# A fused attention and two-layer MLP kernel on one core: weight remainders in halves and at other places, and attention stages in another order

## The reference

```python
# q, k, v: (4 batches, 8 heads, 576, 64)
q_d, k_d, v_d = means over groups of 4 positions
out_up = repeat(softmax(q_d k_d^T / 8) v_d, 4)
out_local = softmax(where(|i - j| < 4, q k^T / 8, -1e9)) v
x = (out_up + out_local) as (2304 tokens, 512)
x = (silu(x w_gate) * (x w_val)) w_out        # d_ff 1536
y = (relu(x w_in) ** 2) w_out2                # d_ff 2048
```

## Time and profile before

| | |
|---|---|
| runs | 945.2, 943.93, 942.46 us; median 943.93 |
| profiled execution | 945.5 us, its span 943.7 us |
| busy: PE, DVE, ACT, POOL | 915.8, 649.4, 403.7, 225.8 us |
| mean granted TensorE clock | 0.982 |
| attention alone | until 53.4 us |
| slots 0 to 47 with pass 0 | 53.4 us to about 242 us |
| passes 1 to 5 begin at | about 282, 421, 562, 704, 846 us |

### The profile page before, as it was taken

The page is one execution under the profiler, slowest core; times in us unless marked ns, Lnnn a source line. Parts: engine busy times, 40 slices in busy tenths (PEclk is TensorE's granted clock), DMA queues, the critical chain, the costliest instruction groups (busy, mean ns, idle before and its releaser), DMA issues.

```text
span 943.7 us, 17134 instructions
## 1 busy us (share of the span) xinstructions
PE 915.8 (97%) x6704; PEld 881.8 (93%) x6704; DVE 649.4 (69%) x1110; ACT 403.7 (43%) x733; POOL 225.8 (24%) x279
## 2 busy tenths in 40 slices
PE   6889999999999999999999999999999999999998
PEld 4678998998999999989999989999999999999998
DVE  6557555655287847696747598666788666778775
ACT  2445454545246443536443535232435232435231
POOL 5575454544242100231100133000323000302000
PEclk8589999999999999999999999999999999999999
DMA  6553333322231111321031121000232010211422
GB/s 198 174 175 93 104 91 103 105 68 73 81 113 49 53 34 34 96 87 49 30 108 53 60 90 67 1 18 17 82 101 71 17 51 17 79 59 54 135 68 67
DMA packets 70880, 71.36 MB, mean 76 GB/s; under 512 B 27280, under 2 KB 58000, under 8 KB 70800
## 3 DMA queue, kind: packets, MB, share of 16 engines
q1 hardware_dynamic: 68496, 65.55, 22.8%
q10 hardware_dynamic: 2304, 4.72, 1.3%
HBM read 56.10 MB, written 14.16 MB: 74 GB/s over the span
## 4 chain that ended last, share of the span: by engine, by line
PE 80%; DVE 9%; ACT 5%; issue 2%; SPq 1%; POOL 1%; DMA 0%; ACTq 0%; DVEq 0%
PE mlp_ps L929 11%; PE mlp_ps L930 10%; PE mlp_ps L931 10%; PE sc L929 5%; PE sc L930 5%; PE sc L931 5%; PE xp L930 4%; PE xp L929 4%; PE xp L931 4%; PE tr L788 3%; PE sd L929 2%; PE sd L931 2%; PE sd L930 2%; PE sc L769 2%; PE tr L929 2%
## 5 line engine op out<-in xcount | busy, mean ns | idle before, releaser
L1309 ACT ACTIVATE wh_hi<-hbuf 128x384 fp32r<-128x384 f32 x144 | 72.4, 524 | 85.4 <-DVE hbuf L1595 61.0
L689 POOL TENSOR_TENSOR w_raw<-w_raw 128x256 f32<-128x256 f32 x16 | 16.7, 1045 | 355.8 <-DMA w_raw<-w_in 355.8
L1603 DVE TENSOR_TENSOR wh_lo<-hbuf,wh_hi 128x384 fp32r<-128x384 f32 x144 | 76.0, 560 | 24.1 <-ACT wh_hi L1309 20.6
L1558 DVE TENSOR_TENSOR ring<-ring_raw,ring 128x768 fp32r<-128x768 f32 x96 | 90.3, 963 | 0.0
L1258 ACT ACTIVATE ring<-ring_raw 128x768 fp32r<-128x768 f32 x96 | 75.3, 836 | 28.9 <-DVE ring_raw L1552 28.6
L929 PE MATMUL mlp_ps<-ring,w_hi 128*128 128x384 f32 x240 | 80.6, 336 | 2.5 <-DVE vbuf L1571 1.9
L931 PE MATMUL mlp_ps<-ring,w_lo 128*128 128x384 f32 x240 | 80.2, 334 | 0.0
L930 PE MATMUL mlp_ps<-ring,w_hi 128*128 128x384 f32 x240 | 80.2, 334 | 0.0
L929 PE MATMUL mlp_ps<-wh_hi,w_hi 128*128 128x384 f32 x216 | 73.2, 339 | 2.6 <-DVE wh_lo L1603 1.5
L930 PE MATMUL mlp_ps<-wh_lo,w_hi 128*128 128x384 f32 x216 | 72.2, 334 | 0.0
L931 PE MATMUL sc<-wh_hi,w_lo 128*128 128x384 f32 x216 | 72.2, 334 | 0.0
(11 more groups left out here) (201 smaller groups left out, 2715.1 us busy)
## 6 DMA issues: line engine op xcount, KB each, us to landing
ring_raw<-x_whole SPq DMA_DIRECT2D x24, 384.0 KB, 3.6
ring_raw<-y_whole SPq DMA_DIRECT2D x24, 384.0 KB, 3.6
qk_sb<-qT SPq DMA_DIRECT2D x16, 288.0 KB, 2.9
qk_sb<-kT SPq DMA_DIRECT2D x16, 288.0 KB, 3.2
v_grp<-v SPq DMA_DIRECT2D x32, 144.0 KB
x_whole<-x_f ACTq DMA_DIRECT2D x16, 288.0 KB, 2.7
y_whole<-ypart SPq DMA_DIRECT2D x3, 1536.0 KB, 5.7
v_win<-v SPq DMA_DIRECT2D x64, 64.0 KB, 2.6
```

The costliest lines, as they stand in the source:

```text
L689: nc.gpsimd.tensor_tensor(block(5), block(7), block(4), ALU.add).then_inc(s_usum[i], 1)
L1309: nc.scalar.activation(hi[:, f, t, :], hbuf[:, e, :], ACT.Copy).then_inc(s_shhi, 1)
L1558: nc.vector.tensor_tensor(ring[:, SLOTS[g][p], 1, :, :], whole(g, p), ring[:, SLOTS[g][p], 0, :, :].bitcast(F32), ALU.subtract).then_inc(s ...
L1603: nc.vector.tensor_tensor(lo[:, f, t, :], hbuf[:, e, :], hi[:, f, t, :].bitcast(F32), ALU.subtract)\
```

## The change

- `SPLIT_IN`, `SPLIT_BEHIND` and `SPLIT_NEXT` become tables for ACT (`HI_...`) and for DVE (`LO_...`); DVE's name halves of a unit, and `LO_SUM` is a further place on DVE, between `dve_c11` and the hidden values of a group in the pass's first chunk.
- Product 2 of a new unit waits only for the first half of its remainder, product 5 for the second.
- Units 0 and 1 of the gated passes swap places in the weight buffer, and pass 0's first tile moves with them. Unit 0 of pass 3 then takes the place of unit 0 of pass 2, which is free earlier.
- Pass 0: DVE's stage 3 goes ahead of stage 7, save in the last slot of a batch. In a batch's first slot the last k step of both tiles comes behind the rest, and ACT's copy of the transposed local probabilities comes ahead of silu. The output tiles m = 0 and m = 1 are run in the order (0,0) (0,1) | (0,2) (1,0) | (1,1) (1,2) | (0,3) (1,3) over the four parts of two slots (tile, hidden tile), and DVE copies both out in the second slot.

```diff
-SPLIT_IN = {2: {2: [0], 3: [1]}, 3: {3: [0]}, 4: {2: [0]}, 5: {2: [0]}}
-SPLIT_BEHIND = {3: [1], 4: [1], 5: [1]}
-SPLIT_NEXT = {1: {0: [2], 1: [3]}, 2: {0: [2], 1: [3]}, 3: {0: [2]}, 4: {0: [2]}, 5: {}}
+HI_IN = {2: {2: [0]}, 3: {2: [0]}, 4: {2: [0]}, 5: {2: [0]}}
+HI_BEHIND = {2: [1, 2], 3: [1, 2], 4: [1, 2], 5: [1]}
+HI_NEXT = {1: {1: [3]}, 2: {0: [3]}}
+LO_IN = {2: {2: [(0, 0), (0, 1)]}, 3: {2: [(0, 0), (0, 1)]}}
+LO_BEHIND = {4: [(0, 0), (0, 1), (1, 0), (1, 1)], 5: [(0, 0), (0, 1), (1, 0), (1, 1)]}
+LO_SUM = {2: {0: [(1, 0), (1, 1)]}, 3: {0: [(1, 0), (1, 1)], 1: [(2, 1)]}, 4: {1: [(2, 1)]}}
+LO_NEXT = {1: {0: [(2, 0), (2, 1)], 1: [(3, 0), (3, 1)]}, 2: {0: [(2, 0), (2, 1)], 1: [(3, 0), (3, 1)]},
+           3: {0: [(2, 0)]}, 4: {0: [(2, 0)]}}
...
-UNITS = [[("in", f, [3072, 0, 1024, 2048][f], 2 * KT * P) for f in range(NF[0])]
+UNITS = [[("in", f, [5376, 0, 1024, 2048][f], 2 * KT * P) for f in range(NF[0])]
...
-    return ([5376, 3584, 0, 1792] if gated(ps) else [3584, 0, 1792])[i]
+    return ([3584, 5376, 0, 1792] if gated(ps) else [3584, 0, 1792])[i]
...
         def pe_mlp(pe, it, cp, j, part):
...
+            starts_batch = j == 0 and cp == 0 and it > 0
+            if j < NF[0] and not starts_batch:
+                pe_first_in(pe, it, cp, j, part, 0, KT)
+            elif j == 0:
+
+                pe_first_in(pe, it, cp, 0, part, 0, KT - 1)
+                if part:
+                    for tile in range(2):
+                        pe_first_in(pe, it, cp, 0, tile, KT - 1, KT)
+            elif it < BATCH - 1 and j < NF[0] + 2:
+
+                for m, f in (((0, 0), (0, 1)), ((0, 2), (1, 0)), ((1, 1), (1, 2)), ((0, 3), (1, 3)))\
+                        [2 * (j - NF[0]) + part]:
+                    pe_first_out(pe, it, cp, m, f, f + 1)
...
-            if c == 0 and p == 2:
-                pe.wait_ge(s_ulo[j], 2 * units_up_to(ps, j))
+            if c == 0 and p in (2, 5):
+
+                pe.wait_ge(s_ulo[j], 2 * units_up_to(ps, j) - (p == 2))
...
         def dve_slot(d, g):
+
+            ends_batch = g % BATCH_SLOTS == BATCH_SLOTS - 1
+            if not ends_batch:
+                for i in pairs_in(3, g):
+                    dve_normalise_loc(d, i)
             for i in pairs_in(7, g):
                 dve_sum_branches(d, i)
...
+            if c == 0:
+                for i, k in LO_SUM.get(ps, {}).get(j, []):
+                    dve_unit_lo(d, ps, i, k)
```

More of the change, by code:

```diff
@@ L933, in pe_mlp, with pe_first_in @@
         def pe_mlp(pe, it, cp, j, part):
-            order = bank_order(it)
+            starts_batch = j == 0 and cp == 0 and it > 0
[10 more added lines that the diff above has]
+                    pe_first_out(pe, it, cp, m, f, f + 1)
+            else:
+                pe_first_out(pe, it, cp, j - NF[0], part * NF[0] // 2, (part + 1) * NF[0] // 2)
+        def pe_first_in(pe, it, cp, j, part, k0, k1):
             c = 2 * it + cp
-            if j < NF[0]:
+            _, _, a, _ = UNITS[0][j]
+            pos = 2 * j + part
+            if k0 == 0:
                 if c == 0:
                     pe.wait_ge(s_firstlo[j], 1)
-                _, _, a, _ = UNITS[0][j]
-                pos = 2 * j + part
                 wait_bank(pe, it, cp, pos)
[L942 to L947, removed]
+            for k in range(k0, k1):
+                if j == 0 and part == 0:
+                    pe.wait_ge(s_xlo, 2 * (PAIRS * it + k) + cp + 1)
+                last = split_products(mlp_bank(it, pos), a + (k * 2 + part) * P,
+                                      (xin[:, x_slot(it, cp), 0, k, :], xin[:, x_slot(it, cp), 1, k, :]),
+                                      k == 0, k == KT - 1)
+            if k1 == KT:
                 last.then_inc(s_in if part else s_gate, 1)
-            else:
-                pe_first_out(pe, it, cp, j - NF[0], part * NF[0] // 2, (part + 1) * NF[0] // 2)
         def pe_first_out(pe, it, cp, m, f0, f1):
@@ L1176, in act_slot @@
                 act_move_ds(a, i, 1)
+            starts_batch = g > 0 and g % BATCH_SLOTS == 0
+            if starts_batch:
+                for i in pairs_in(4, g):
+                    act_move_loc1(a, i)
             act_mlp(a, *mlp, "gate")
@@ L1182, in act_slot @@
             for i in pairs_in(4, g):
-                act_move_loc1(a, i)
+                if not starts_batch:
+                    act_move_loc1(a, i)
                 act_move_loc2(a, i)
@@ L1366, in act_chunk @@
             if c == NC - 1 and ps + 1 < PASSES:
-                for i in SPLIT_BEHIND.get(ps + 1, []):
+                for i in HI_BEHIND.get(ps + 1, []):
                     act_unit_hi(a, ps + 1, i)
@@ L1495, in dve_slot @@
                 dve_maximum_ds(d, i)
-            for i in pairs_in(3, g):
-                dve_normalise_loc(d, i)
+            if ends_batch:
+                for i in pairs_in(3, g):
+                    dve_normalise_loc(d, i)
             for i in pairs_in(4, g):
@@ L1517, in dve_mlp @@
                 m = j - NF[0]
-                d.wait_ge(s_out, MT + out_tile(c, m) + 1)
-                nc.vector.tensor_copy(ypart_at(c, m), out_bank(it, m)).then_inc(s_y, 1)
+                for t in {0: [], 1: [0, 1]}.get(m, [m]) if it < BATCH - 1 else [m]:
+                    d.wait_ge(s_out, MT + out_tile(c, t) + 1)
+                    nc.vector.tensor_copy(ypart_at(c, t), out_bank(it, t)).then_inc(s_y, 1)
         def dve_hidden_lo(d, gi, lo, B, hi):
@@ L1638, in dve_group @@
             if c == NC - 1 and ps + 1 < PASSES:
-                for i in SPLIT_IN[ps + 1].get(j, []):
-                    dve_unit_lo(d, ps + 1, i)
+                for i, k in LO_IN.get(ps + 1, {}).get(j, []):
+                    dve_unit_lo(d, ps + 1, i, k)
             if c == 0:
-                for i in SPLIT_NEXT[ps].get(j, []):
-                    dve_unit_lo(d, ps, i)
+                for i, k in LO_NEXT.get(ps, {}).get(j, []):
+                    dve_unit_lo(d, ps, i, k)
         def dve_y(d, g, i):
@@ L1693, in dve_chunk @@
             if c == NC - 1 and ps + 1 < PASSES:
-                for i in SPLIT_BEHIND.get(ps + 1, []):
-                    dve_unit_lo(d, ps + 1, i)
+                for i, k in LO_BEHIND.get(ps + 1, []):
+                    dve_unit_lo(d, ps + 1, i, k)
             dve_y(d, g, 7)
@@ L1700, in dve_last_batch @@
             if cp == 0 and j == 4:
-                dve_unit_lo(d, 1, 0)
+                for k in range(2):
+                    dve_unit_lo(d, 1, 0, k)
             if cp == 0 and j == 5:
@@ L1720, in dve_last_batch @@
             if cp == 1 and j == 5:
-                dve_unit_lo(d, 1, 1)
+                for k in range(2):
+                    dve_unit_lo(d, 1, 1, k)
         def dve_mask(d):
```

18 lines of the change are left out of this document (8 added, 10 removed).

## The result

| | before | changed |
|---|---|---|
| runs beside each other, median | 943.74 us of 4 | 956.37 us of 4 (951.54 to 957.12) |
| ratio | | 1.0121, 95% interval 1.0093 to 1.0148 |
| profiled execution, its span | 945.5, 943.7 us | 957.12, 955.3 us |
| mean granted TensorE clock | 0.982 | 0.980 |

The changed kernel is slower, as forecast, but by 11.4 us by the ratio (by its interval 8.8 to 14.0; the two medians are 12.6 apart), where the sum said 6.2. It ends above the forecast's range, whose upper end was 954.5. A second session timed the same kernel at 954.05 against 944.54 of the kernel before (1.0101, 1.0085 to 1.0118), so 9 to 13 us are to be explained.

The account below looks back on a forecast made before the run. PE, busy 97% of the span, was taken as the bound. Parts 1 to 3 add 11.9 and part 4 takes off 5.75: +6.2 on 943.9 gives 950.1 us; the sum's ends are 945 and 953, the range 943.5 to 954.5.

Parts of the forecast that it names:

- Part 1: Pass 0, DVE normalises before summing: slots 11 to 35 lose 4 x 1.38, slots 7, 23, 39 lose 3 x 0.73.
- part 2: Batch starts, slots 16 and 32: transposition starts no earlier, three matmuls now behind it, 0.4 more each, 0.8.
- Rivals 1 and 2: Pass 0: ACT's chain stays hidden, 936.0, chance 0.08; or only branch-sum waits and batch starts cost, 939, chance 0.06.
- Slots 3 and 43: Pass 0, late coarse normalising: slot 3 loses 1.5 (1.3 to 1.8), slot 43, without slack, loses 1.9.
- Part 3: Pass 0, output tiles' new order: last hidden tile used some 2.5 us later, nothing further to count.
- Part 4: Pass changes, weight units' remainders moved: 5.75 us less in all, bounds 4 to 7.
- The same at the end of pass 2: Unit 0's remainder goes a group earlier there: gain 1.5, as at the end of pass 1.
- First groups of passes 3 and 4: PE's pauses there come from both halves of unit 2's remainder; moving one behind gains 0.7 each, 1.4.
- rival 3: As forecast, but moved remainders also late, at product 2 of passes 4 and 5 and first groups: +2.4, 952.5, chance 0.12.
- The first 60 us: Kernel start, where attention runs alone: only a place in memory changes, so no time gained or lost.

Follow-up runs that it names:

- gate_first: The changed kernel with ACT's gate silu ahead of the splits of x in slots 3, 11, 19, 27, 35 and 43: 941.21 us, ratio 0.9972.
- tiles_old: The changed kernel with output tiles 0 and 1 again in the old order, each copied out in its own slot: 954.31 us, ratio 1.0121.
- after_again: The changed kernel run once more with no edit: 954.05 us, ratio 1.0101 to the kernel before.
- lo21_back: Kernel before with only the new remainder tables and swapped places, unit 2's second half again in group 0 of passes 3 and 4: 938.39 us.
- pool_late: Kernel before with only the new remainder tables and swapped places, POOL's next-unit sums held back at the ends of passes 1 and 2: 942.22 us.
- gate_plain: lo21_back with ACT's gate silu first in slots 3, 11, 19, 27, 35 and 43: 937.83 us, ratio 0.9933.
- gate_tiles: gate_plain with the changed kernel's order of output tiles 0 and 1 besides: 939.99 us, ratio 0.9953.

## Why the prediction was wrong in its size

- **Part 1, slots 11 to 35 and 7, 23, 39; part 2: right.** 4 x 1.38 + 3 x 0.73 + 2 x 0.4 = 8.5 forecast, 4 x 1.28 + 2.4 + 0.8 = 8.3 measured, by the mechanism named. At the batch start the transposition starts no earlier and three matmuls stand behind it, as said. Rivals 1 and 2, in which this chain is hidden, have fallen with gate_first.
- **Slots 3 and 43, "I take 1.5" and 1.9: mis-sized, the largest error.** The chain alone costs 2.0 (tiles_old) and 1.8 (after_again). Behind pauses this long PE's clock fell to half, another 1.2 in slot 43; slot 3 shows 1.5 more, the fall and 0.3 or so of the tiles' order together. The sum had a pause's length and its refill and no price for the clock: 3.4 for the two slots against 6.5 in the profiled execution and 5.3 in the second.
- **Part 3, the output tiles, at nothing: right**, within 0.3 in slot 3 and nothing elsewhere. It names other waits (w_lo, buf_b, probsT_l), and the sum of the pauses stays.
- **Part 4, 5.75 less: too large, by 1.75.** "The same at the end of pass 2: 1.5" failed most: that end gave 0.4. The pause ahead of it went as forecast (1.2 with its refill), but the wait for wh_lo grew from 0.36 to 0.62, as POOL's sums stood beside both of DVE's products, and the wait for ypart behind it from 0.54 to 1.04, as POOL's sum there started ahead of DVE's copy. I had used the trace's 1.62 for two products beside POOL, and took pass 2's end to be like pass 1's. "First groups of passes 3 and 4, 0.7 each ... from both halves of unit 2's remainder, of which one is moved behind" failed in its cause and then in its size: by lo21_back the 0.4 that is gained comes from ACT's hi part being ready earlier, and moving the half gives 0.3 more and takes it back a group later. That is my rival 3 in kind (the moved remainders late), but not in place: at product 2 of passes 4 and 5, where I looked for it, nothing waits.
- **The first 60 us, at nothing.** The profiled execution of the changed kernel lost 0.9 there, its second gained 0.6: the execution's, not the change's.

Sum, of the profiled execution: 0.9 + (14.8 - 11.9) + (5.75 - 4.0) = 5.5, and its span is longer by 11.6, where the forecast had 6.2. In after_again it is -0.6 + 13.6 - 3.5 = 9.5, as its span is longer by 9.5. Both parts erred the same way, so no error hid another. (One slip besides: the chances of rivals 1 and 2 add up to 0.14, and "faster" was given 0.13.) By its sign and chain the forecast was right; its upper end of 953, in the sum, held no case in which a long pause costs more than itself.

## To carry to other kernels

Before an in-order engine's idle wait is filled with other work, list who waits for the work that used to fill it: here DVE's branch sums were ACT's ticket to the splits and the silu queued behind them, and putting silu first in that queue gave back 11 us by the steps of pass 0 (13 by the medians). In this kernel a pause of 2 to 3 us on a busy PE cost its length and, five times in eight, a stretch at half clock worth 1.2 to 1.4 us more; such a chance belongs in the sum. And an instruction moved out of a pause lands somewhere else; ask which engine works beside it there.

## What the hardware showed that I had not expected

- The half clock behind pauses of 2 to 3 us in all: in eight such places five had it and three did not, and slot 44 of the changed kernel had it in one execution of two. Each time it lasted 3.4 us, and cost 1.2 to 1.4 between like programs. Behind the single pauses of 1.9 us in pool_late (at 418.94 and 558.40) it stayed at 1.00.
- POOL beside DVE: with an operation of POOL on SBUF at work, DVE's products of 128x384 take up to 1.10 us (with two operands from SBUF) and 1.84 (`SCALAR_TENSOR_TENSOR`) in place of 0.55, and the remainder 1.09 in place of 0.56. Who starts first decides who is drawn out: at pass 2's end POOL's sum of 128x256 takes 0.74 to 0.86 when it starts ahead of DVE's 128x768 (which then takes 1.50 to 1.53; in pool_late POOL, 0.45 ahead, took 1.14), and 1.18 to 1.43 when it starts behind it (DVE 0.95).
- By this, executions of one and the same program differ at the ends of passes 1 and 2. At pass 1's end the wait for wh_lo is 0.74 to 0.79 in the four executions (after_again, lo21_back, gate_plain, gate_tiles) where POOL's second sum starts 0.01 to 0.17 us ahead of DVE's first product, and 0.21 or 0.22 in the six where it starts level with it or behind. At pass 2's end it is the wait for ypart, 0.5 more or less (above). POOL starts when its weights have landed, so by the traces the landing of that load decides; no run moved it.
- The first 60 us are not the same from one execution to the next, whatever the kernel. PE starts the values of the fourth pair at 46.6 to 52.7 us in the 13 profiled executions of this study, and it is at half clock for 13.7 to 34.1 us in all before 62 us. The two go together: with 13.7 us at half clock slot 2's values start at 64.1 and 64.7, with 20.5 at 65.5 to 66.5, with 23.9 at 67.2, with 27.3 to 34.1 at 68.5 to 70.2. That is more than most edits here are worth. Why an execution falls on one side stays open.
